# One distance table for all heads, queries scaled on GpSimd, and the first weights split there too, in an attention and gated feed-forward kernel

## The reference

```python
rel = pos[:, None] - pos[None, :]
is_global = pos[None, :] < n_global                    # 8
is_local = (rel >= 0) & (rel < n_local)                # 96
dist = where(is_global & ~is_local, n_local, abs(rel))
slopes = 2.0 ** (-8.0 * (arange(H) + 1) / H)
scores = q @ k.T / 8 - slopes * dist                   # -1e9 where neither global nor local
x = softmax(scores) @ v                                # heads side by side: (B, S, 512)
h = relu(x @ w_in); y = (h * sigmoid(conv3(h))) @ w_out          # 512 -> 1024 -> 512
z = relu(y @ w_in2); u, v = z[..., :512], z[..., 512:]
out = (u * (w_spatial @ layernorm(v) + b_spatial)) @ w_out2
```

## Time and profile before

| | before |
|---|---|
| median of 3 runs | 374.99 us (374.44 to 375.29) |
| the profiled execution | 374.08 us |
| its span, first to last instruction | 372.0 us |
| busy: PE, DVE, ACT, POOL | 97%, 58%, 47%, 20% |
| first f1 product starts at | 34.56 us |

### The profile page before, as it was taken

One profiled execution on the slowest core, in us unless ns is written; L12 is line 12 of the kernel. 1 busy time (PEld: TensorE's weight loads), 2 busy tenths in 40 slices (PEclk: granted clock), 3 DMA queues, 4 the chain that ended last, 5 costly groups with the idle time before them and its releaser, 6 DMA issues.

```text
span 372.0 us, 6143 instructions
## 1 busy us (share of the span) xinstructions
PE 361.2 (97%) x2266; PEld 323.9 (87%) x2266; DVE 214.7 (58%) x568; ACT 176.6 (47%) x450; POOL 76.2 (20%) x152
## 2 busy tenths in 40 slices
PE   6798999999999999999999999999999999999995
PEld 3466888888888899999988999998899999998884
DVE  5798586767677678679957690213863444441000
ACT  4798575674756469664255650213563111112121
POOL 4859963223233100000020210001410000000000
PEclk9999999999999999999999999999999999999999
DMA  7923323142302304131100000001141000001322
GB/s 234 409 112 130 102 86 127 35 154 84 125 37 70 131 0 169 62 112 56 58 0 0 3 0 0 2 0 45 56 168 60 0 2 0 0 2 58 114 86 90
DMA packets 11796, 27.69 MB, mean 74 GB/s; under 512 B 1520, under 2 KB 3568, under 8 KB 11760
## 3 DMA queue, kind: packets, MB, share of 16 engines
q1 hardware_dynamic: 11328, 26.95, 20.6%
q10 hardware_dynamic: 432, 0.28, 0.2%
HBM read 24.08 MB, written 3.15 MB: 73 GB/s over the span
## 4 chain that ended last, share of the span: by engine, by line
PE 91%; ACT 3%; DVE 3%; DMA 1%; POOL 1%; issue 1%; DVEq 0%; ACTq 0%
PE bank L1502 19%; PE bank L1504 19%; PE bank L1503 19%; PE bank L1471 19%; PE bank L1447 5%; PE bank L1425 4%; PE bank L1404 4%; ACT p_sb L683 2%; DMA counts<-in_n_keys 1%; DVE p_sb L1004 1%; DVE denom L1013 0%; POOL p_sb L588 0%; DVE dist L980 0%; ACT pt_sb L691 0%; POOL bias L576 0%
## 5 line engine op out<-in xcount | busy, mean ns | idle before, releaser
L1471 PE MATMUL bank<-xT,w_hi 128*128 128x384 f32 x256 | 71.3, 348 | 0.0
L588 POOL TENSOR_SCALAR p_sb<-p_sb,denom 128x256 f32<-128x256 f32 (+1 forms) x96 | 44.3, 481 | 53.3 <-DVE denom L1015 53.1
L1471 PEld LDWEIGHTS bank<-xT,w_hi 128*128 128x128 f32 x256 | 45.6, 188 | 3.5 <-issue 2.5
L683 ACT ACTIVATE p_sb<-p_sb,row_min 128x256 f32<-128x256 f32 (+1 forms) x96 | 46.3, 486 | 2.2 <-DVE row_min L1004 2.0
L1471 PE MATMUL bank<-xT,w_lo 128*128 128x384 f32 x128 | 44.6, 348 | 0.0
L1502 PE MATMUL bank<-g_hi,w_hi 128*128 128x386 f32 (+1 forms) x128 | 43.3, 338 | 0.0
L1504 PE MATMUL bank<-g_hi,w_lo 128*128 128x386 f32 (+1 forms) x128 | 43.2, 337 | 0.0
L1503 PE MATMUL bank<-g_lo,w_hi 128*128 128x386 f32 (+1 forms) x128 | 43.1, 337 | 0.0
L1041 DVE SCALAR_TENSOR_TENSOR c_sb<-h_sb,conv_sb,c_sb 128x382 f32<-128x382 f32 (+1 forms) x64 | 40.2, 628 | 2.3
L691 ACT COPY pt_sb<-bank 128x512 f32<-128x512 f32 (+1 forms) x41 | 22.6, 552 | 36.7 <-PE bank L1425 36.7
L1004 DVE CUSTOM_DVE_ANT_0 p_sb<-bank,bias 128x256 f32<-128x256 f32 (+1 forms) x96 | 33.1, 399 | 3.6 <-PE bank L1404 2.9
(11 more groups left out here) (96 smaller groups left out, 750.4 us busy)
## 6 DMA issues: line engine op xcount, KB each, us to landing
stage<-in_weights SPq DMA_DIRECT2D x17, 512.0 KB, 3.2
v_sb<-in_v SPq DMA_DIRECT2D x8, 390.0 KB, 3.1
k_sb<-in_k SPq DMA_DIRECT2D x8, 384.0 KB, 3.4
out_dram<-out_sb SPq DMA_DIRECT2D x12, 256.0 KB, 2.0
q_sb<-in_q SPq DMA_DIRECT2D x14, 192.0 KB, 2.5
k_sb<-in_k SPq DMA_DIRECT2D x6, 256.0 KB, 3.4
v_sb<-in_v SPq DMA_DIRECT2D x5, 260.0 KB, 2.7
stage_late<-in_weights SPq DMA_DIRECT2D x2, 512.0 KB, 12.5
```

Source lines behind the costliest of these rows:

```text
L588: nc.gpsimd.tensor_scalar(probs_h, probs_h, denom[:, u % SLOTS, h:h + 1], 1.0, ALU.mult, ALU.mult).then_inc(scaled, 1)
L683: nc.scalar.activation(p_sb[:, u % SLOTS, h, 0:n], p_sb[:, u % SLOTS, h, 0:n], ACT.Exp, bias=row_min[:, u % SLOTS, h:h + 1], scale=-1.0, a ...
L1471: last = nc.tensor.matmul(banks[5 + j % 3][:, 0:C], w, x, start=r == 0, stop=r == F1_GROUP - 1)
```

## The change

What it does:
- Scores are no longer biased by a table of their own head. There is one `table`; POOL multiplies the queries by 1 / (slope times 2^38) with a column of constants `q_scale` (eight small memsets on DVE), and the bias instruction's scale multiplies slope times 2^38 back.
- DVE builds the table in three parts of 128, 256 and 256 columns, each just ahead of its first use. The eight multiples on DVE, ACT and POOL are gone.
- POOL scales the queries of triple 0 in two parts and of triple 1 before its first unit, of triples 2 and 3 behind unit 1, and of each later triple pg behind unit 3*pg//2*2 - 7, which is 5, 7, 11, 13, 17 and so on. PE waits for `q_scaled` in place of the queries' arrival.
- POOL splits all of the first weights, in eight pieces, behind the units 11, 13, 15, 16, 18, 19, 21 and 22. ACT and DVE split none of them.
- The second pair of score banks is used for pairs up to unit 16 (DOUBLED = 18), by the pairs 0, 4, 8, 12, 16. `f1` waits for the bias of unit 17 and, only at its third group, for the copy of unit 13.
- DVE biases units 4 and 5 before it inverts the sums of units 2 and 3.
- The first loads are cut: queries of triple 0 in two, its keys in two, the first of them on ACT's queue; the values of triple 0 and the convolution weights move from ACT's queue to SP's.

```diff
+PIECE_UNITS = (11, 13, 15, 16, 18, 19, 21, 22)
+DOUBLED = F1_FIRST + 4
...
         def score_bank(u, h):
-            if u < F1_FIRST and u // 2 % 2:
+            if u < DOUBLED and u // 2 % 2 == 0:
                 return banks[5 + h]
...
+        def queries_scaled(pg, tt):
+            if pg == 0:
+                return 1 if tt < 2 else 2
+            return pg + 2 if pg < 2 else max(pg, 3) + 1
+        def scale_unit(pg):
+            return TG * pg // 2 * 2 - 7
...
         def _(sp):
...
-                if n == NW1:
-                    sp.wait_ge(w1a_split, 2)
-                if n == NW1 + 1:
-                    sp.wait_ge(w1_split, PIECES)
+                if n in (NW1, NW1 + 1):
+                    sp.wait_ge(w1_split, PIECES * (n - NW1 + 1))
...
-            sp.dma_start(q0_sb[:, 0, :], q[0]).then_inc(q_first, 16)
-            sp.dma_start(k0_sb[:, 0, :], k0[0]).then_inc(k_first, 16)
+            sp.dma_start(q0_sb[:, 0, 0:2 * P], q[0, :, 0:2 * P]).then_inc(q_first, 16)
+            sp.dma_start(q0_sb[:, 0, 2 * P:C], q[0, :, 2 * P:C]).then_inc(q_third, 16)
+            sp.dma_start(k0_sb[:, 0, 2 * P:K0W], k0[0, :, 2 * P:K0W]).then_inc(k_third, 16)
...
+            sp.dma_start(v0_sb[:, 0, :], v0[0]).then_inc(v_first, 16)
...
+            sp.dma_start(conv_sb[:], conv_w).then_inc(conv_in, 16)
...
         def _(pool):
...
-            def table(n):
...
+            pool.wait_ge(slopes_in, 2 * HP)
+            def scale_queries(pg):
+                queries = q_sb[:, pg % 2, :]
+                pool.wait_ge(q_in[pg % 2], 16 * (pg // 2 - 1))
+                nc.gpsimd.tensor_scalar(queries, queries, q_scale[:, pg % HP:pg % HP + 1], 1.0, ALU.mult, ALU.mult
+                                        ).then_inc(q_scaled, 1)
...
+            scale_first_queries(0, slice(0, 2 * P), q_first, True)
+            scale_first_queries(0, slice(2 * P, C), q_third, True)
+            scale_first_queries(1, slice(0, C), q_second, True)
...
-            for n in range(2, 4):
-                table(n)
             for u in range(ALL_UNITS):
                 scale_probs(u)
-                if u in (1, 2, 4, 5):
-                    table(4 + u // 2 + u // 5)
-                if PIECE_FIRST <= u < PIECE_FIRST + (NW1 - 1) * PIECES:
-                    split_piece(u - PIECE_FIRST)
+                if u == 1:
+                    scale_first_queries(2, slice(0, C), q_rest, False)
+                    scale_first_queries(3, slice(0, C), q_rest, True)
+                for pg in range(HP, ALL_TRIPLES):
+                    if scale_unit(pg) == u:
+                        scale_queries(pg)
+                if u in PIECE_UNITS:
+                    split_piece(PIECE_UNITS.index(u))
...
         def _(act):
-            act.dma_start(v0_sb[:, 0, :], v0[0]).then_inc(v_first, 16)
-            act.dma_start(conv_sb[:], conv_w).then_inc(conv_in, 16)
+            act.dma_start(k0_sb[:, 0, 0:2 * P], k0[0, :, 0:2 * P]).then_inc(k_first, 16)
...
-                if u in (6, 8):
-                    round_half(u // 2 - 3)
...
         def _(dve):
...
+            for hp in range(HP):
+                for h in range(2):
+                    nc.vector.memset(q_scale[h * D:(h + 1) * D, hp:hp + 1], -SCALE / (slope(2 * hp + h) * UNIT)
+                                     ).then_inc(slopes_in, 1)
...
+            def build_table(at_col, width):
+                cols, near = slice(at_col, at_col + width), table[:, at_col:at_col + GK]
+                link(nc.vector.scalar_tensor_tensor(table[:, cols], rel[:, cols], nl, behind[:, cols], ALU.is_ge,
+                                                    ALU.max))
+                link(nc.vector.tensor_tensor(near, near, reach[:], ALU.min))
...
-                        in1=bias[:, 2 * hp + h, at_col:at_col + n],
-                        scale=-SCALE, scalar=FAR, op0=ALU.add, op1=ALU.min,
+                        in1=table[:, at_col:at_col + n],
+                        scale=slope(2 * hp + h) * UNIT, scalar=FAR, op0=ALU.add, op1=ALU.min,
...
-            for h in range(2):
-                link(nc.vector.tensor_scalar(bias[:, h, AT_T0:TW], dist[:, AT_T0:TW], slope8(h) * UNIT, None, ALU.mult))
+            build_table(AT_T0, P)
             bias_scores(0)
-            dve.wait_ge(table_of_0, 1)
-            dve.wait_ge(table_of_1, 1)
+            build_table(AT_T1, 2 * P)
             bias_scores(1)
             invert_sums(0, 1)
+            build_table(AT_LATER, 2 * P)
             bias_scores(2)
             invert_sums(1, 1)
             bias_scores(3)
+            bias_scores(4)
+            bias_scores(5)
...
-                if u in (7, 9):
-                    rest_of_half((u - 7) // 2)
...
         def _(pe):
...
-                        pe.wait_ge(q_in[slot], 16 * (pg // 2 - 1))
+                        pe.wait_ge(q_scaled, queries_scaled(pg, tt))
...
-                wait_if(pe, biased, 2 * u - (4 if u < F1_FIRST else 0))
+                wait_if(pe, biased, 2 * u - (4 if u <= DOUBLED else 0))
...
-                if u >= F1_FIRST:
+                if u == F1_FIRST:
+                    wait_pt(pe, u - 2)
+                if u > F1_FIRST:
                     wait_pt(pe, u - 1)
-                    wait_pt(pe, u - 2)
...
-                    pe.wait_ge(biased, 2 * F1_FIRST)
+                    pe.wait_ge(biased, 2 * DOUBLED)
+                if i == 2 * F1_GROUP:
                     wait_pt(pe, F1_FIRST - 1)
...
-                    if kappa == 0 and m == 0:
-                        pe.wait_ge(w1a_split, 2)
-                    if kappa == 0 and m >= 2 and m % 2 == 0:
-                        pe.wait_ge(w1_split, PIECES * (m // 2))
+                    if kappa == 0:
+                        pe.wait_ge(w1_split, m + 1)
```

More of the change, by code:

```diff
@@ L176, in build_program @@
         att = Packer("c1")
-        bias = att("bias", [P, H, TW])
+        table = att("table", [P, TW])
+        q_scale = att("q_scale", [P, HP])
         q_sb = att("q_sb", [P, 2, C])
@@ L573, in _, with scale_first_queries @@
                                     pattern=[[-1, P]], channel_multiplier=1).then_inc(consts, 1)
-            def table(n):
[L576 to L581, removed]
+            pool.wait_ge(slopes_in, 2 * HP)
[4 more added lines that the diff above has]
+                                        ).then_inc(q_scaled, 1)
+            def scale_first_queries(hp, cols, semaphore, done):
+                queries = q0_sb[:, hp, cols]
+                pool.wait_ge(semaphore, 16)
+                last = nc.gpsimd.tensor_scalar(queries, queries, q_scale[:, hp:hp + 1], 1.0, ALU.mult, ALU.mult)
+                if done:
+                    last.then_inc(q_scaled, 1)
+            scale_first_queries(0, slice(0, 2 * P), q_first, True)
+            scale_first_queries(0, slice(2 * P, C), q_third, True)
+            scale_first_queries(1, slice(0, C), q_second, True)
             def scale_probs(u):
@@ L592, in split_piece @@
             def split_piece(i):
-                n, part = divmod(i + PIECES, PIECES)
+                n, part = divmod(i, PIECES)
                 cols = slice(part * PIECE, (part + 1) * PIECE)
@@ L671, in split_hi @@
                 nc.scalar.copy(hi, staged(chunk)[:, 0:hi.shape[-1]]).then_inc(w_rounded, 1)
[L673 to L677, removed]
             def soften(u):
@@ L757, in _ @@
             nc.scalar.activation(spare[:], minus_half[:], ACT.Exp, bias=minus_half[:], scale=-1.0)
-            act.wait_ge(tables, DIST_STEPS)
-            nc.scalar.activation(bias[:, 0, 0:AT_T0], dist[:, 0:AT_T0], ACT.Copy, scale=slope8(0) * UNIT
-                                 ).then_inc(table_of_0, 1)
             for u in range(4):
@@ L979, in _ @@
             link(nc.vector.tensor_scalar(count_f[:, 6:7], nl, 1.0 / UNIT, None, ALU.mult))
-            link(nc.vector.scalar_tensor_tensor(dist[:, 0:TW], rel[:], nl, behind[:], ALU.is_ge, ALU.max))
             link(nc.vector.tensor_scalar(reach[:], key[:], ng, count_f[:, 6:7], ALU.is_ge, ALU.add))
-            near = dist[:].rearrange("p (t n) -> p t n", n=2 * P)[:, :, 0:GK]
-            link(nc.vector.tensor_tensor(near, near, reach[:], ALU.min))
-            assert steps[0] == DIST_STEPS, steps[0]
+            def build_table(at_col, width):
[3 more added lines that the diff above has]
+                link(nc.vector.tensor_tensor(near, near, reach[:], ALU.min))
             def path_tests():
@@ L998, in bias_scores @@
                 at_col = (AT_T0, AT_T1, AT_LATER)[min(t, 2)]
-                if g == 0 and tt == 0:
-                    wait_if(dve, later_tables, 2 * hp)
                 wait_if(dve, turned, u + 1 - SLOTS)
@@ L1136, in _ @@
                     invert_sums(u + 2, 2)
-                if u % 2 == 0 and u + 4 < ALL_UNITS:
+                if u % 2 == 0 and 0 < u and u + 4 < ALL_UNITS:
                     bias_scores(u + 4)
```

42 lines of the change are left out of this document (14 added, 28 removed).

## The result

The changed kernel took 377.46 us (376.03 to 379.14 in nine runs) against 374.99 for the kernel before (373.77 to 376.02 in nine): a ratio of 1.0079, 95% interval 1.0055 to 1.0103. It is slower, by about 2.5 to 3 us, where 1.55 was forecast, which is 0.7 to 0.8%. The profiled execution took 377.46 with a span of 375.7, 3.7 more than before.

The account below looks back on a forecast made before the run. PE bounds the kernel, so the end moves with the first f1 product: 2.2 us won, 3.75 lost, f1 1.55 later. Added to 374.08 that gives 375.6 for a profiled execution, 376.5 for the median; range 374.3 to 378.2.

Parts of the forecast that it names:

- First scores, table, early units: In the start, PE begins at 5.45 us, 0.8 sooner; later table parts take 0.6 each; unit 4's bias at 11.1, not 12.56.
- PE's pace: After scores of units 8 and 9, PE sets the pace; scores of 14 and 15 end at 25.65, 1.4 sooner.
- The wait that is moved into POOL's queue: Behind unit 11, POOL waits for triple 6's queries until 28.0, delaying piece 0 and scales 12 and 13; 3.75 us lost.
- scale 14: 35.85; its last transposes: 36.1, and f1 starts: End of POOL's chain: unit 14 scaled by 35.85 us, f1 starting at 36.1 in place of 34.56, 1.55 later.
- the idle time of about 1 us that was forecast ahead of unit 14: Sign in the changed profile: PE idle again about 1 us ahead of unit 14's transposes, with POOL named.
- What was costed at nothing: Behind the start, POOL's extra pieces and scalings, later query loads, memsets, f1's waits and later issues were taken to cost nothing.
- the lead of 1.6: POOL's margin over PE during f1: unit 20 scaled near 52.4 us, needed at 54, so PE never stops.
- the small hole after 40 us: PE was to have no hole after f1 starts; holes after 40 us would show the prediction wrong.
- POOL starves f1: Rival: the lead at unit 20 is missing as POOL's instructions stretch beside DVE; 1 to 2 us more, 378; chance 0.07.
- The port: Rival: DVE and POOL hold each other up in the first 15 us; 0.7 later, 377.2; chance 0.12.
- The rival on the other side: Rival: the query load hides and POOL doesn't stand at unit 11; f1 at 32.35, 2.2 sooner, 372.8; chance 0.12.

Follow-up runs that it names:

- the last experiment: Version with queries scaled one turn later and zeros in PE's first holes, bias of units 4 and 5 put back behind sums of 2 and 3: 372.84 us.
- the first experiment: Changed kernel with every later query scaling one PE turn later on POOL (triple 6 behind unit 13, not 11): 374.22 us, ratio 0.9972.

## Why the prediction was right

The forecast was 376.5 us within 374.3 to 378.2, slower with a chance of 0.70. It took 377.46. That the median is only 0.96 above the forecast is partly luck: for the profiled execution the forecast was 375.6, and that took 377.46, 1.9 more. The step from the one to the other, 0.91, was taken from a profiled execution of the kernel before that was faster than its median; that of the changed kernel was its median. The start of f1 was forecast 1.55 later than before and came 2.27 later.

**First scores, table, early units: right.** PE started at 5.55 (forecast 5.45), DVE's first bias at 6.63 (6.55), unit 4's bias at 11.26 (11.1). The table parts took 0.48 and 0.47, with 0.19 and 0.24 for the minima, for which 0.45 and 0.15 had been taken.

**PE's pace: right.** The scores of 14 and 15 ended at 25.49 for a forecast of 25.65. The gain of 1.4 was 1.57. Of it, the early bias of units 4 and 5 is about half (0.7 in the last experiment's profile).

**The wait that is moved into POOL's queue: right**, in place and in size. Query scaling started at 28.00 (28.0), the scales of 12 and 13 ended at 32.33 (32.4), that of unit 14 at 35.7 (35.85). The scalings took 0.58 each (0.56), the load 2.5 rather than 2.3. Two experiments confirm it from two sides: the scaling moved, or the load made early, brings the distance to f1 from 11.34 to 7.40 and 7.76.

**What PE does behind the hole: missed.** The step "scale 14: 35.85; its last transposes: 36.1, and f1 starts" supposed that PE, having waited, would be back at POOL's heels at its old speed. It had to weigh and score at half the clock, and came to unit 14 at 36.42, later than POOL, whose first scale of that unit had ended near 35.3. So the idle time of about 1 us that was forecast ahead of unit 14 wasn't there, and the one ahead of unit 12 was 2.74 for about 2. This term of the sum was 0 and measured 0.87 in the profile.

**What was costed at nothing: one item wrong.** The sentence was that the queries of triple 8 and later have a whole slower turn more to land in. They had, and it wasn't enough: POOL stood 1.20 us for those of triple 8 and 1.94 for those of triple 9. It ended unit 20 at 54.5 for the 52.4 of the forecast, and the lead of 1.6 was gone. The count also stopped at unit 20, and two more pieces follow, behind 21 and 22. PE waited for unit 23, the small hole after 40 us that the prediction had named as a sign of being wrong, and 0.75 us went. The rival "POOL starves f1" had the place, one to two units of work too early, and about twice the price, but named the stretching of POOL's instructions as the reason. They did stretch, as it said, though they do so as well in the version with the scaling moved (1.53 at 42.83), where PE doesn't wait; from POOL's timeline of the changed kernel:

```profile
46.99 1.53 POOL L612 TENSOR_SCALAR p_sb<-p_sb,denom 128x256 f32<-128x256 f32 x2
```

Two scales that take 0.93 elsewhere took 1.53 here, while DVE's tap instructions (L1058, 687 ns in the mean for 628 before) ran beside them.

**The sum.** 1.57 won, and 3.0 lost to the queue, 0.87 to the clock, 0.75 to the starved turns: that is 3.05, and PE's last product comes 3.04 later than before. The other 0.6 or so between the spans is the tail behind it.

**The port: not seen in the table parts.** The two later ones took 0.48 and 0.47, the first with POOL idle and the second beside POOL's scales of unit 0, from 9.09 on. The add of units 2 and 3, at 0.41 us for 0.17, was held again, this time by the scaling of the queries. By the rule of the Trainium skill, "SBUF — State Buffer", section "SBUF: two separate sides", that is what should happen to it, and the stretched pairs above would be the same lock seen from POOL. For the adds the traces agree. In the first 75 us of the changed kernel four of them took 0.30 to 1.25 us, and each ended 0.02 to 0.03 us after an instruction of POOL (13.05 for 13.02, 34.85 for 34.82, 41.48 for 41.46, 53.60 for 53.57). With a piece moved beside it, another went from 0.17 to 1.15. For the stretched pairs no run separated the lock from other causes.

**The rival on the other side** would have been 372.8, if POOL had not stood at unit 11. It is the kernel of the first experiment, whose f1 starts at 33.02 for the 32.35 of this rival, and where its clock held it took 372.3 to 372.7.

## What to carry to other kernels

When an operand gets one more step on another engine, ask when that operand arrives and what stands behind the step in that engine's queue. A load that was hidden for its reader isn't hidden for whoever must touch it first, and an in-order engine passes the wait on to work that has nothing to do with it. The place that is late enough for the load and early enough for the reader was one turn later, and it turned a loss of 2.5 us into a time that is 0.8 below the kernel before, a difference that the interval just about allows (0.9972, 0.9945 to 1.0000).

## What the runs showed of the hardware that was not expected

A hole in PE costs more than its length. After 2.74 us of idle time the granted clock fell to 0.50 for about 3 us, and 0.87 us went on top; all nine executions of the changed kernel have a mean clock of 0.983 to 0.995. Shorter holes in a row (1.64, 1.17 and 0.77 us within 6 us) are followed by a stretch at 0.50 in some profiles and not in others. With such holes filled by zeros (1.42, 1.17 and 0.77 us in its profile) the executions of one kernel went from 372.3 to 375.3 to 371.6 to 373.4, all at 0.997 of the clock or more.

A small instruction on DVE can take some seven times its usual time beside POOL. The add of 128x4 to the sums takes 0.17 us, and took 1.15 and 1.25 where it began just behind the start of the second half of a piece on POOL (1.27 and 1.46 us).

The query scaling one turn later with the zeros in the first holes is at 0.9952 (0.9938 to 0.9966) of the kernel before, so it beats both; with the banks single as well it is the same within the intervals (0.9939, 0.9916 to 0.9961).
